# Attention and two MLPs on one core: partial sums of the seven w_out products kept in PSUM banks instead of in u2 and u3

## What is computed

```python
def reference(q, k, v, cap, moe_w_in, moe_w_out, moe2_w_in, moe2_w_out):
    # q, k, v: (2, 12, 448, 64)
    scores = cap * tanh(q @ k.T / 8 / cap)
    attn = softmax(scores) @ v                  # to x: 896 tokens x 768
    g = maximum(x @ moe_w_in, 0) ** 2           # 896 x 2048
    x = g @ moe_w_out                           # 896 x 768
    h = x @ moe2_w_in
    return (h * sigmoid(h)) @ moe2_w_out        # 896 x 768
```

## Time and profile before

| what | before |
| --- | --- |
| median of 3 runs | 532.4 us (532.32 to 532.47) |
| profiled execution, span from first to last instruction | 530.5 us |
| TensorE busy | 521.6 us, 98% |
| VectorE busy | 363.4 us, 69%, 627 instructions |
| ScalarE busy | 261.1 us, 49% |
| granted TensorE clock, mean over the span | 0.999 |

### The profile page before, as it was taken

How to read it: one execution, slowest core, us unless ns; L and a number is a source line. 1 busy time by engine, 2 the same in 40 slices (tenths; PEclk the granted TensorE clock), 3 DMA queues, 4 the chain that set the end, 5 groups by cost and what they waited for, 6 DMA issues and landing times.

```text
span 530.5 us, 7104 instructions
## 1 busy us (share of the span) xinstructions
PE 521.6 (98%) x2628; PEld 440.2 (83%) x2628; DVE 363.4 (69%) x627; ACT 261.1 (49%) x404; POOL 77.5 (15%) x52
## 2 busy tenths in 40 slices
PE   7999999999999999999999999999999999999996
PEld 5333334799999999999999999999999999999996
DVE  3388888797778644677789845556865345568986
ACT  4999997155444322444445344454533144454330
POOL 1999999000000000000000000000000000000000
PEclk9999999999999999999999999999999999999999
DMA  8799611152202202422021025202121241020546
GB/s 221 193 241 226 179 44 32 29 140 59 80 0 80 59 2 59 140 59 65 15 80 39 22 61 139 61 14 67 41 65 34 61 138 34 27 80 2 122 69 97
DMA packets 82181, 42.17 MB, mean 79 GB/s; under 512 B 26848, under 2 KB 79072, under 8 KB 82144
## 3 DMA queue, kind: packets, MB, share of 16 engines
q1 hardware_dynamic: 77984, 40.32, 29.7%
q10 hardware_dynamic: 4128, 1.38, 1.1%
q0 software_dynamic: 32, 0.00, 0.0%
HBM read 38.93 MB, written 2.75 MB: 79 GB/s over the span
## 4 chain that ended last, share of the span: by engine, by line
PE 95%; ACT 3%; issue 1%; DVE 1%; POOL 0%; ACTq 0%; POOLq 0%
PE banks L557 27%; PE banks L558 27%; PE banks L559 27%; PE banks L477 4%; PE banks L470 4%; PE banks L498 2%; PE banks L467 1%; ACT prob L690 1%; ACT prob L683 1%; PE banks L524 1%; PE banks L489 1%; DVE asum L924 0%; ACT prob L680 0%; DVE den_s L916 0%; POOL cap_b L421 0%
## 5 line engine op out<-in xcount | busy, mean ns | idle before, releaser
L557 PE MATMUL banks<-x_hi,w_hl 128*128 128x448 f32 x384 | 139.5, 363 | 0.0
L558 PE MATMUL banks<-x_lo,w_hl 128*128 128x448 f32 x384 | 138.8, 362 | 0.0
L559 PE MATMUL banks<-x_hi,w_hl 128*128 128x448 f32 x384 | 138.7, 361 | 0.0
L557 PE MATMUL banks<-g_hi,w_hl 128*128 128x448 f32 (+1 forms) x340 | 122.8, 361 | 0.0
L559 PE MATMUL banks<-g_hi,w_hl 128*128 128x448 f32 (+1 forms) x340 | 122.3, 360 | 0.0
L558 PE MATMUL banks<-g_lo,w_hl 128*128 128x448 f32 (+1 forms) x340 | 122.1, 359 | 0.0
L557 PEld LDWEIGHTS banks<-x_hi,w_hl 128*128 128x128 f32 x384 | 72.1, 188 | 6.1 <-issue 1.4
L559 PEld LDWEIGHTS banks<-x_hi,w_hl 128*128 128x128 f32 x384 | 71.9, 187 | 5.3
L558 PEld LDWEIGHTS banks<-x_lo,w_hl 128*128 128x128 f32 x384 | 71.9, 187 | 4.4
L982 DVE TENSOR_TENSOR w_hl<-w_raw,w_hl 128x768 fp32r<-128x768 f32 x32 | 31.9, 997 | 55.4 <-ACT w_hl L716 55.3
L559 PEld LDWEIGHTS banks<-g_hi,w_hl 128*128 128x128 f32 x340 | 63.8, 188 | 4.6
(11 more groups left out here) (68 smaller groups left out, 526.4 us busy)
## 6 DMA issues: line engine op xcount, KB each, us to landing
w_raw<-in_moe_w_in_dram SPq DMA_DIRECT2D x32, 384.0 KB, 3.4
w_raw<-in_moe_w_out_dram SPq DMA_DIRECT2D x24, 512.0 KB, 5.3
qk_raw<-in_k_dram SPq DMA_DIRECT2D x44, 112.0 KB, 3.3
qk_raw<-in_q_dram SPq DMA_DIRECT2D x44, 112.0 KB, 3.3
v_t<-in_v_dram SPq DMA_DIRECT2D x24, 96.0 KB, 3.3
out_dram<-rows SPq DMA_DIRECT2D x38, 56.0 KB, 2.2
qk_raw<-in_k_dram ACTq DMA_DIRECT2D x4, 112.0 KB, 3.2
qk_raw<-in_q_dram ACTq DMA_DIRECT2D x4, 112.0 KB, 4.2
```

The source lines that it names most:

```text
L557: pe.matmul(dst, hi[:, kk, :], mov_hi, start=start, stop=False, skip_group_check=onto)
L558: pe.matmul(dst, hi[:, kk, :], mov_lo, start=False, stop=False, skip_group_check=onto)
L559: return pe.matmul(dst, lo[:, kk, :], mov_hi, start=False, stop=stop, skip_group_check=onto)
```

## The change

The products come in another order, P1, P5, P6, P2, P7, P3, P4, and go into three banks: P1, P6, P7, P4 one after the other onto bank 0, P5 and P3 onto bank 1, P2 into bank 2. After each of them the running sum of the bank is read and added to y by one addition (`take` on VectorE); at s=0 the first reads of a y tile and the read after P4 are copies on ScalarE (`y_copy`). The sign of `t4` is turned, so P4 is added. u2, u3, `p1_copy` and `s_p1` are gone. Onto a bank nothing may be accumulated before its sum so far is read, so TensorE waits for the read after product 0 before product 2, after product 2 before product 4, and after product 4 before product 6. In the last group of the program the last product goes, in its two parts, into banks that are free. Both kernels' TensorE queues have the same matmuls. In `hidden` the first tile of layer 1 takes the x tiles in a slightly changed order, in which they now come.

```diff
-        MOVING = (G_B11, G_T1, G_T2, G_T3, G_B21, G_B22, G_T4)
+        G_B11, G_T1, G_T2, G_B21, G_T3, G_B22, G_T4 = range(NP)
-        BANK_OF = (0, 3, 1, 2, 0, 3, 1)
+        BANK_OF = (0, 1, 0, 2, 0, 1, 0)
+        ONTO = (2, 4, 5, 6)
+        Y_AFTER = (0, 1, 2, 0, 1, 2, 3)
@@ TensorE, model
-                elif n == 4:
-                    pe.wait_ge(s_p1, group_no(layer, s, g) + 1)
-                elif n == 5 and s == 0:
-                    pe.wait_ge(s_y_act, y_copies(layer, g, 1))
-                elif n == 5:
-                    pe.wait_ge(s_post, post(layer, s, g, 1))
-                elif n == 6:
-                    pe.wait_ge(s_post, post(layer, s, g, 1 if s == 0 else 2))
+                elif n in (2, 4, 5):
+                    taken = (1, 3, 2)[(2, 4, 5).index(n)]
+                    if s == 0:
+                        pe.wait_ge(s_y_act, y_copies(layer, g, taken))
+                    else:
+                        pe.wait_ge(s_post, post(layer, s, g, taken))
+                elif n == 6 and not (layer == 1 and s == 1 and g == GROUPS - 1):
+                    pe.wait_ge(s_post, post(layer, s, g, 2 if s == 0 else 5))
@@ ScalarE
-            def p1_copy(layer, s, g):
+                        if g > 0 and s == 0:
+                            y_copy(layer, g - 1, 6)
+                        if s == 0:
+                            y_copy(layer, g, 0)
...
@@ VectorE
-            def post_u2(layer, s, g):
-            def post_u3(layer, s, g):
...
+            def take(layer, s, g, n):
+                made(layer, s, g, n)
+                if s == 1 and n in (3, 4, 5):
+                    dve.wait_ge(s_post, post(layer, s, g, n - 2))
+                add(y_of(g, Y_AFTER[n]), y_of(g, Y_AFTER[n]), y_bank(g, BANK_OF[n])).then_inc(s_post, 1)
...
+                    take(layer, s, 0, 3)
+                    take(layer, s, 0, 4)
+                    prod_low(layer, s, 0, 6)
+                    t4(layer, s, KQ - 1)
+                    g_low(layer, s, KQ - 1, G_T4)
+                    prod_low(layer, s, 1, 0)
+                    w_s1(layer, s, 1)
+                    w_s3(layer, s, 1)
+                    w_s2(layer, s, 1)
+                    prod_low(layer, s, 1, 1)
+                    leave(layer, s, 0, 0)
+                    leave(layer, s, 0, 1)
+                    take(layer, s, 0, 5)
+                    if s == 1:
+                        prod_low(layer, s, 1, 2)
+                    for g in range(1, GROUPS):
...
+                        if s == 1:
+                            take(layer, s, g - 1, 6)
+                        if s == 0 or g > 1:
+                            prod_low(layer, s, g, 2)
+                        w_s4(layer, s, g)
+                        leave(layer, s, g - 1, 2)
+                        if s == 1:
+                            take(layer, s, g, 0)
+                        prod_low(layer, s, g, 3)
```

More of the change, by code:

```diff
@@ L584, in hidden @@
                 fresh = layer == 1 and s == 0 and p == 0
-                order = [(kk, b) for kk in (0, 3, 1, 4, 2) for b in range(B)] + [(5, 1), (5, 0)]
+                order = [(kk, b) for kk in (0, 3, 1, 4) for b in range(B)] + [(2, 0), (5, 1), (2, 1), (5, 0)]
                 for n, (kk, b) in enumerate(order):
                     if fresh:
-                        ready = 4 * (n // 4) + (2, 3, 1, 4)[n % 4] if n >= 8 else 4 * (n // 4 + 1)
+                        ready = n + 1 if n >= 8 else 4 * (n // 4 + 1)
                         pe.wait_ge(s_x, PAIRS + ready)
@@ L634, in model @@
                                   g_hi[:, q, kk, :], g_lo[:, q, kk, :],
-                                  kk == 0 and n not in (4, 5), kk == KQ - 1, n in (4, 5))
+                                  kk == 0 and n not in ONTO, kk == KQ - 1, n in ONTO)
                 last.then_inc(s_prod, 1)
@@ L785, in _ @@
                     for p in range(SF):
+                        if p == 0 and s == 1:
+                            y_copy(layer, GROUPS - 1, 6)
                         if p == 0 and layer == 1 and s == 0:
@@ L845, in _ @@
                             x_high(g, 1)
+                        if g == 0 and s == 1:
+                            prod_high(layer, s, 1, 2)
+                        if x_too and g < GROUPS - 1:
+                            x_high(g, 2)
             def store(m, b, a, t=slice(0, QB)):
@@ L1058, in odd_chunk @@
                 t3(layer, s, i)
-                for q in (G_T2, G_T3, G_B21):
+                for q in (G_T2, G_B21, G_T3):
                     g_low(layer, s, i, q)
@@ L1132, in turn_rows @@
                 m, b = y_tile(g, n)
-                posted(1, 1, g, after)
+                dve.wait_ge(s_post, post(1, 1, g, after))
                 dve.transpose(rows[m][:, b, :], y[:, m, b, :]).then_inc(s_rows, 1)
@@ new lines, in _ @@
+                    prod_low(layer, s, 0, 1)
+                    if layer == 0:
+                        relu_squared(s, SF - 1)
+                    if s == 1:
+                        take(layer, s, 0, 0)
+                    prod_low(layer, s, 0, 2)
+                    t2(layer, s, KQ - 1)
+                    g_low(layer, s, KQ - 1, G_T2)
+                    prod_low(layer, s, 0, 3)
+                    g_low(layer, s, KQ - 1, G_B21)
+                    prod_low(layer, s, 0, 4)
+                    t3(layer, s, KQ - 1)
@@ new lines, in _ @@
+                    if s == 1:
+                        take(layer, s, 0, 1)
+                        take(layer, s, 0, 2)
+                    w_s4(layer, s, 0)
+                    g_low(layer, s, KQ - 1, G_T3)
+                    prod_low(layer, s, 0, 5)
+                    g_low(layer, s, KQ - 1, G_B22)
+                    take(layer, s, 0, 3)
[3 more added lines that the diff above has]
+                    g_low(layer, s, KQ - 1, G_T4)
@@ new lines, in _ @@
+                    prod_low(layer, s, 1, 0)
[9 more added lines that the diff above has]
+                    for g in range(1, GROUPS):
+                        last = g == GROUPS - 1
+                        end = last and layer == 1 and s == 1
+                        if s == 1:
+                            take(layer, s, g - 1, 6)
[3 more added lines that the diff above has]
+                        leave(layer, s, g - 1, 2)
+                        if s == 1:
+                            take(layer, s, g, 0)
+                        prod_low(layer, s, g, 3)
+                        leave(layer, s, g - 1, 3)
@@ L1237, in _ @@
-                        if g > 0:
-                            if s == 1:
-                                post_12_u2(layer, g)
-                            if not last:
-                                w_s1(layer, s, g + 1)
-                        post_u3(layer, s, g)
-                        if last and layer == 1 and s == 1:
-                            post_22(layer, s, g)
-                            turn_rows(g, 0, 5)
-                            prod_low(layer, s, g, 6)
-                            post_11(layer, g)
-                            turn_rows(g, 1, 6)
-                            post_21_u3(layer, g)
-                            post_12(layer, s, g)
-                            break
@@ L1268, in _ @@
-                        if g == 1:
+                        if not last:
+                            w_s1(layer, s, g + 1)
+                        take(layer, s, g, 3)
+                        if end:
+                            leave(layer, s, g, 0)
+                        prod_low(layer, s, g, 6)
+                        take(layer, s, g, 4)
+                        if end:
+                            add(y_of(g, 3), y_of(g, 3), y_bank(g, BANK_OF[4])).then_inc(s_post, 1)
+                            leave(layer, s, g, 1)
+                            take(layer, s, g, 5)
+                            break
@@ L1269, in _ @@
+                        if not last:
                             prod_low(layer, s, g + 1, 0)
-                        if s == 1:
-                            post_11(layer, g)
                         leave(layer, s, g, 0)
-                        if g == 1:
+                        if not last:
                             w_s3(layer, s, g + 1)
-                        if g == 1:
                             w_s2(layer, s, g + 1)
                             prod_low(layer, s, g + 1, 1)
-                        elif last and s == 0:
+                        elif s == 0:
@@ L1280, in _ @@
                             tile_low(layer, 1, 0)
-                        elif last and layer == 0:
+                        elif layer == 0:
                             tile_low(1, 0, 0)
-                        post_12(layer, s, g)
-            leave(1, 1, GROUPS - 1, 2)
+                        leave(layer, s, g, 1)
+                        take(layer, s, g, 5)
+            turn_rows(GROUPS - 1, 2, 7)
             m, b = y_tile(GROUPS - 1, 3)
-            posted(1, 1, GROUPS - 1, 7)
             for part, cols in enumerate(LAST_COLS):
```

173 lines of the change are left out of this document (40 added, 133 removed).

## The result

The changed kernel takes 535.25 us (median of 4 runs, 535.04 to 535.51), before 532.43 beside it: a ratio of 1.0053, 95% interval 1.004 to 1.0065. It is slower by 2.8 us; 535.3 was forecast.

A forecast was written before the change was run, and what follows sets the result against it. TensorE alone was taken to bound the kernel from 97 us on; two stalls of 1.53 us less 0.15 repaid gave +2.9 us on 532.4, so 535.3 us, range 533.9 to 536.7.

The forecast's parts named there:

- TensorE alone sets the time: From 97 us on: matmuls of model and hidden have 0.0 us idle before them, so only new TensorE waits cost time.
- What is removed: 23 VectorE post-additions, 12.4 us less work, worth 0 directly; a late weight load at g=0 product 6 repays 0.15 us.
- The waits in free places cost nothing: Where the reader stands free, a read ends 0.81 us into the next product's 2.40, 1.6 us to spare.
- The seam: From g=0 to g=1, both s=1 stages: product 2 waits for VectorE's read after product 0; 1.53 us lost each.
- the seventeen pitches: VectorE start-to-start times from read after g=0's product 4 through g=1's read after product 0, its length included; 10.77 us.
- the release: At g=1 product 2, s=1: TensorE's weight load follows 0.04 us after the end of VectorE's read.
- The restart: After a waited-for weight load the second matmul comes after 0.32 us, not 0.20; 0.12 us more per stall.
- Nothing is passed on to g=2: After either stall VectorE has three short pieces before product 3, then waits for TensorE again; no further loss.
- the tail: Program end: last two part additions start on TensorE's release, last product goes into two unheld banks; change zero.
- Not slower: Rival: g=1's bank 0 read after product 0 comes in time after all, 1.41 us earlier; 532.25 us; chance 0.09.
- more places: Rival: other products stall, nearest product 4 of g=0 at s=1, which holds by 0.6 us; 536.4 to 538; chance 0.08.
- The falling clock: Rival: clock halves after each stall, 540 to 545 us; chance 0.04; against it, clock 1.00 in 28:32 despite 0.64 us idle.

The follow-up runs named there:

- reads first: Changed kernel with w_s4 and three departures of y tiles moved behind VectorE's bank 0 read after product 0, from g=0 into g=1 at s=1; 532.17 us, again 532.17.
- ScalarE reads: Changed kernel, but at g=1 of both s=1 stages ScalarE copies bank 0 after product 0 and VectorE adds the copy; 532.27 us.
- own bank: Changed kernel, but at g=1 of both s=1 stages products 2, 4, 6 use free bank 3, leaving P1 out of three y tiles; 532.14 us.
- one piece more: Changed kernel plus one 128x448 scratch addition in VectorE's queue before g=1's first bank 0 read, both s=1 stages; 537.09 us, again 537.99 us.
- three pieces more: Changed kernel plus three scratch additions in VectorE's queue before g=1's first bank 0 read, in both s=1 stages; 541.82 us.

## Why the prediction was right

**TensorE alone sets the time: right.** Its busy time and matmuls stayed, and taking both stalls away (reads first, ScalarE reads, own bank) gives 532.1 to 532.3 three times.

**What is removed: right.** VectorE lost 11.9 us of busy time (12.4 forecast) and this was worth nothing; the late weight load at product 6 of g=0 is gone. Overlooked was the second late load, at product 3 of g=1, which is gone too: 0.23 us repaid in all, not 0.15.

**The waits in free places cost nothing: right.** The view of waits from 97 us on has none of the new waits of the s=0 stages, none of g=0 and g=2 at s=1, and at g=1 only the one before product 2.

**The seam: right, with one step of it mis-sized.** The sum of the seventeen pitches was 10.77 us, counted from the start of read 4; in the rows it is 282.14 - 271.38 = 10.76. The lateness at which read 0 ends was forecast as 1.37 us behind product 2's due time and is 1.36 (282.14 against 280.78). Mis-sized was the release: 0.04 us from the end of VectorE's instruction to TensorE's weight load, taken from a load that waits for split weights. Behind the read the load starts 0.12 us later (282.14 to 282.26) and the matmul 0.15. The restart was right: from this load to the second matmul 0.31 us (282.26 to 282.57), against 0.32. So the stalls cost 1.59 and 1.56 us instead of twice 1.53, 0.09 more together, and 0.08 more was repaid by weight loads than forecast. That the sum of 2.91 us meets the 2.92 between the first and the last matmul is luck to this extent: two errors of 0.1 us cancelled.

**Nothing is passed on to g=2, and the tail: right.** The last part addition still stands on TensorE's release and starts 0.31 us behind the start of the last matmul, 528.96, as it does in the earlier trace rows behind 525.91:

```profile
529.27 0.35 DVE L1060 TENSOR_TENSOR y<-y,banks 128x192 f32<-128x192 f32 x1 [0.42 <-PE banks L559]
```

**The rivals.** Not slower and more places did not come. The falling clock did not come in the changed kernel either, but I had it too far away: the row of 28:32 that I set against it has a pause of at most 0.64 us and says nothing of longer ones. The pauses here are 1.5 us, and at 2.0 us (one piece more) the clock fell in five of eight runs: 0.5 us was between the forecast and a time up to 3.5 us higher. Its price I had too high: in the trace a fall took nine matmuls and 1.6 us, where I had set one or two products and 2.4 to 4.8. The Trainium skill, TensorE: Matmul & The Clock Gate, section "A second HAM failure mode: psum-queue depth-cycling", tells of a kernel whose clock goes up and down because of short pauses between its groups of matmuls. The trace of three pieces more agrees that such a pause can let the clock fall (0.75 in 285:290), though there are only two of them, 221 us apart; the pauses of the changed kernel, too, lie between groups of matmuls, and none of its nine runs shows a fall.

## What to carry to other kernels

Where partial sums are chained in one PSUM bank, each read gets a deadline of one product; lay the reader's queue out from the deadline back, and put what only leaves (splits of results, transposes, weight sums that are wanted later) behind the read. An engine at two thirds of its time can still be the one that is waited for, at the single place where its queue is full, and making it work less elsewhere changes nothing. This queue was priced to 0.1 us by adding up the pitches of the trace before; its first piece was tied to a moment that can't move, the end of a product.

## What was not expected of the hardware

TensorE's clock fell to the lower level after pauses that are short. With matmuls 2.24 us from start to start across the pause, some executions of the same program show a fall by their time and granted clock and others don't (536.3, 538.0 or 539.9 us); with 3.3 us the profiled one shows it at both seams; with 1.7 us it came in none of nine runs. In the trace the first fall is there at once behind the pause and the second 1.3 us after TensorE was at work again; each cost about 1.6 us. And the weight load that waits for VectorE's read started 0.12 us behind the read's end, its matmul 0.15, where the load that waits for a split started 0.04 us behind that.
